# Fused attention and two expert layers: layer two of a token tile issued behind layer one of the next tile, and all transposes of a tile in one block of 64-row turns

## The reference

```python
def _moe2_ref(x, w_gate, w_output_gate, w1, w2):
    logits = x @ w_gate
    e_idx = np.argmax(logits, axis=1)
    ...
    for e in range(E):                      # E = 8
        mask = e_idx == e
        if not mask.any():
            continue
        h = np.maximum(x[mask] @ w1[e], 0.0)      # 512 -> 1024
        ye = h @ w2[e]                            # 1024 -> 512
        out[mask] = gate_w[mask, None] * eom[mask, e, None] * ye
```

## Time and profile before

| | |
|---|---|
| runs | 889.3, 894.98, 890.36 us; median 890.36 |
| the profiled execution | 894.22 us, of which the span from the first to the last instruction is 892.5 us |
| busy share of the span | PE 96%, DVE 43%, ACT 29%, POOL 18% |
| mean granted TensorE clock | 0.991 of full speed |
| chain that ended last | PE 90%, DVE 3%, issue 3%, DMA 2% |

### The profile page before, as it was taken

How to read it: one execution, slowest core, us unless ns; L and a number is a source line. 1 busy time by engine, 2 the same in 40 slices (tenths; PEclk the granted TensorE clock), 3 DMA queues, 4 the chain that set the end, 5 groups by cost and what they waited for, 6 DMA issues and landing times.

```text
span 892.5 us, 18919 instructions
## 1 busy us (share of the span) xinstructions
PE 857.6 (96%) x7096; PEld 720.9 (81%) x7097; DVE 385.5 (43%) x770; ACT 257.1 (29%) x387; POOL 163.7 (18%) x223
## 2 busy tenths in 40 slices
PE   8998998999999999999999999998989999999994
PEld 6897897888888888888888888987768888888883
DVE  5786895211133322334223341467765224534431
ACT  4564453111131112211131111325243113323311
POOL 5775300700000000000000000000133333322321
PEclk9999998999999999999999999999999999999997
DMA  9885733500020000200020000106611116106100
GB/s 260 241 245 171 234 119 104 154 1 0 1 95 1 1 1 0 94 0 0 0 71 0 0 0 0 49 1 213 213 50 46 47 35 221 55 35 229 40 25 18
DMA packets 51301, 68.54 MB, mean 77 GB/s; under 512 B 9774, under 2 KB 36014, under 8 KB 51248
## 3 DMA queue, kind: packets, MB, share of 16 engines
q1 hardware_dynamic: 44400, 45.20, 15.9%
q0 software_dynamic: 6560, 22.56, 7.9%
q10 hardware_dynamic: 288, 0.02, 0.0%
HBM read 54.11 MB, written 14.70 MB: 77 GB/s over the span
## 4 chain that ended last, share of the span: by engine, by line
PE 90%; DVE 3%; issue 3%; DMA 2%; ACT 1%; SPq 0%; DVEq 0%; ACTq 0%; POOL 0%; POOLq 0%
PE bank L1347 32%; PE bank L1366 15%; PE bank L1544 11%; PE bank L1572 11%; PE bank L1318 4%; PE bank L1236 4%; PE bank L1263 4%; PE bank L1559 2%; PE bank L1300 1%; PE bank L1376 1%; PE bank L1509 1%; PE bank L1418 1%; PE bank L1337 1%; DMA xg<-y_rows,early_rows 1%; DMA k_sb<-kT 1%
## 5 line engine op out<-in xcount | busy, mean ns | idle before, releaser
L989 DVE TENSOR_TENSOR prod<-silu,bank 128x512 f32<-128x512 f32 x48 | 33.0, 686 | 182.9 <-PE bank L1347 182.9
L1347 PE MATMUL bank<-x_hi,wg_hi 128*128 128x512 f32 (+1 forms) x240 | 91.5, 381 | 0.0
L1347 PE MATMUL bank<-x_hi,wg_lo 128*128 128x512 f32 (+1 forms) x240 | 88.5, 369 | 0.0
L1347 PE MATMUL bank<-x_lo,wg_hi 128*128 128x512 f32 (+1 forms) x240 | 88.4, 368 | 0.0
L1347 PE MATMUL bank<-x_hi,wv_hi 128*128 128x512 f32 (+1 forms) x240 | 88.3, 368 | 0.0
L1347 PE MATMUL bank<-x_lo,wv_hi 128*128 128x512 f32 (+1 forms) x240 | 88.3, 368 | 0.0
L1347 PE MATMUL bank<-x_hi,wv_lo 128*128 128x512 f32 (+1 forms) x240 | 88.3, 368 | 0.0
L517 POOL DMA_INDIRECT xg<-y_rows,early_rows x2 | 3.0, 1522 | 430.2 <-DVE early_rows L947 429.9
L641 ACT ACTIVATE silu<-bank 128x512 f32<-128x512 f32 x48 | 28.7, 598 | 179.6 <-PE bank L1347 179.6
L1366 PE MATMUL bank<-wo_hi,h_hi 128*128 128x512 f32 x192 | 75.5, 393 | 0.0
L1366 PE MATMUL bank<-wo_hi,h_lo 128*128 128x512 f32 x192 | 74.8, 390 | 0.0
(11 more groups left out here) (244 smaller groups left out, 1621.5 us busy)
## 6 DMA issues: line engine op xcount, KB each, us to landing
e_w<-w SPq DMA_DIRECT2D x32, 512.0 KB, 6.0
stage<-w_out POOLq DMA_DIRECT2D x16, 384.0 KB, 3.9
y_rows<-y_sb SPq DMA_DIRECT2D x18, 256.0 KB, 2.1
k_sb<-kT SPq DMA_DIRECT2D x16, 256.0 KB, 4.9
v_sb<-v SPq DMA_DIRECT2D x16, 256.0 KB, 4.7
q_sb<-qT SPq DMA_DIRECT2D x16, 256.0 KB, 3.5
x_rows<-x_sb SPq DMA_DIRECT2D x16, 256.0 KB, 4.1
x_in<-x_rows SPq DMA_DIRECT2D x4, 1024.0 KB, 5.7
```

The costliest lines, as they stand in the source:

```text
L989: dve.tensor_tensor(both(prod[:]), both(silu[:]), bank[V_BANK][:], ALU.mult).then_inc(prod_ready, 1)
L1347: mm = pe.matmul(acc[:, 0:width], w[:, k, cols], x[:, k, 0:width], start=(k == 0 and i == 0), stop=(k == KC - 1 and i == 2))
```

## The change

Five things change in the expert layer and in its run-up.

1. **The shift.** In PE's loop, layer one of tile `t` is followed by layer two of tile `t-1`. Layer two of the last tile stands behind the loop.
2. **One block of turns.** Between steps 3 and 4 of that layer two, PE transposes all of `h_sb` of tile `t` and the rows of tile `t+1`, in 24 transposes of 64 rows (upper and lower half alternating, into different banks) in place of 12 of 128 rows. Before step 3 it waits for the ReLU and for the gathered rows (`turnable`).
3. **Wider operations.** ACT does the ReLU of all 1024 columns in one operation, and `hT_hi`; DVE `hT_lo`; each 1024 columns wide. DVE's scaling of tile `t-1` (`scaled_ahead`) stands behind `hT_lo` of tile `t`, and `hT_hi` of tile `t` waits until layer two of tile `t-1` is done, since `hT_hi` is a single buffer.
4. **The run-up.** Routing steps of the 256-token group go one or two steps `c` earlier or later; tile 1 gets its own row buffer, so both early gathers are issued together; `choose_first` and `early_places` come earlier.
5. **The tables.** Columns first (`col_ready`), the rest after; `hT_lo` of tile 1 goes ahead of the table; the turn of tile 2's rows goes from step 6 to step 2 of tile 1's layer two; POOL looks up tile 1's scale before it gathers tile 2.

PE:

```diff
             layer2(1, 0, 0, 1)
             turn_h(1, 1)
-            layer2(1, 0, 1, 6)
+            layer2(1, 0, 1, 2)
             turn_rows(2)
-            layer2(1, 0, 6, EC)
+            layer2(1, 0, 2, 4)
...
-            with pe.Fori(2, tiles) as t:
-                rank = pe.value_load(table[0:1, bass.ds(t + T_RANK, 1)], min_val=0, max_val=E - 1)
...
+            def turnable(t):
+
+                pe.wait_ge(ha_ready, t + 1)
+                pe.wait_ge(xg_in, (t + 1) * 16)
+
+            def turn_halves(t):
+
+                for c in range(EC):
+                    for a in range(2):
+                        rows = slice(a * TAIL, (a + 1) * TAIL)
+                        mm = pe.transpose(bank[2 + a][:, c * TAIL:(c + 1) * TAIL], h_sb[rows, c * P:(c + 1) * P], ident[rows, rows])
+                mm.then_inc(ht_done, 1)
...
+            first_layer(2)
+            layer2(1, 0, 4, 5)
+            turnable(2)
+            layer2(1, 0, 5, 6)
+            turn_halves(2)
+            layer2(1, 0, 6, EC)
+            with pe.Fori(3, tiles) as t:
+                first_layer(t)
+                rank = rank_of(t - 1)
+                second_layer(t - 1, rank, 0, EC // 2 - 1)
+                turnable(t)
+                second_layer(t - 1, rank, EC // 2 - 1, EC // 2)
+                turn_halves(t)
+                second_layer(t - 1, rank, EC // 2, EC)
+            second_layer(tiles - 1, rank_of(tiles - 1), 0, EC)
```

ACT and DVE:

```diff
+            def h_high_halves(t):
+
+                act.wait_ge(ht_done, t + 3)
+                act.wait_ge(l2_done, alone(act, t + 1))
+                act.activation(by_halves(hT_hi[:]), h_halves(), ACT.Copy).then_inc(hthi_ready, 1)
+
             with act.Fori(2, tiles) as t:
-                relu(t, 0)
-                h_high(t, 0)
-                rows_high(t + 1)
-                h_high(t, 1)
+                relu_all(t)
+                rows_high_halves(t + 1)
+                h_high_halves(t)
                 share(t)
...
+            def scaled_ahead(u):
+
+                dve.wait_ge(l2_done, u + 1)
+                dve.wait_ge(ro_ready, alone(dve, u))
+                dve.wait_ge(sc_in, u * 16)
+                dve.tensor_scalar(o_sb[:], bank[7][:], scale_in[:, 0:1], None, ALU.mult).then_inc(o_ready, 1)
+
+            rows_low_halves(3)
+            h_low_halves(2)
+            share(2)
+            with dve.Fori(3, tiles) as t:
+                rows_low_halves(t + 1)
+                h_low_halves(t)
+                scaled_ahead(t)
                 share(t)
-                scaled(t)
+            scaled_ahead(tiles)
```

POOL:

```diff
-            early_gather(0)
+            for t in range(TT):
+                early_gather(t)
             pool.wait_ge(early_at_ready, 1)
             pool.wait_ge(scale_out, 16)
             scale_lookup(scale_early, EARLY * P, early_at[:, 0:1])
-            pool.wait_ge(xt_done, 1)
-            early_gather(1)
             scatter(0, early_rows[:, 0:1])
+            scale_lookup(scale_early, EARLY * P, early_at[:, 1:2])
...
             gather_ahead(0)
-            tiles = pool.value_load(table[0:1, T_TILES:T_TILES + 1], min_val=1, max_val=SLOTS)
+            gather_ahead(1)
+            scatter(1, early_rows[:, 1:2])
...
-            with pool.Fori(1, tiles) as t:
+            with pool.Fori(2, tiles) as t:
                 tile(t)
```

More of the change, by code:

```diff
@@ L171, in build @@
         e_lo = sb("e_lo", [P, 2 * CH * CW], F32R)
[L172 to L175, removed]
+        xg, xg_second = stage[:, 0, 0:DM], stage[:, 1, 0:DM]
+        xgT_hi, xgT_lo = (sb(n, [P, KC * P], F32R) for n in ("xgT_hi", "xgT_lo"))
+        hT_hi, hT_lo = (sb(n, [P, EC * P], F32R) for n in ("hT_hi", "hT_lo"))
         h_sb = sb("h_sb", [P, EF])
-        hT_lo = sb("hT_lo", [P, EC * P], F32R)
         o_sb = sb("o_sb", [P, DM])
@@ L847, in route_at @@
             def route_at(g):
-                return (4, 5, 0) if isinstance(g, int) and g == NG - 1 else (R_BANK, R_BANK, 256)
+                return (4, 5, 0) if isinstance(g, int) and g in (NG - 3, NG - 1) else (R_BANK, R_BANK, 256)
             def choose(g, base):
@@ L1137, in _ @@
+            col_t = of_tile(t1[:], shift_e[:], te2)
+            then(next(col_t),
+                 dve.memset(table[0:1, T_COL + SLOTS:T_COL + 32], 0))
+            then(next(col_t))
+            dve.tensor_tensor(table[0:1, T_COL:T_COL + SLOTS], t1[0:1, :], iota_f[0:1, 0:SLOTS], ALU.add
+                              ).then_inc(col_ready, 1)
+            then(dve.tensor_tensor(ee2[:], earlier[:], over_tiles(used_e[:], E), ALU.mult),
                  dve.tensor_tensor(e1[:], used_e[:], iota_f[:, 0:E], ALU.mult),
@@ L1138, in _ @@
                  dve.tensor_tensor(e3[:], used_e[:], base_e[:], ALU.mult))
-            then(dve.tensor_tensor(te_in[:], te_in[:], te1[:], ALU.mult),
+            then(dve.tensor_reduce(rank_e[:], ee2[:], AX.X, ALU.add))
+            scaled(0)
+            rank_t = of_tile(t_rank[:], rank_e[:], te1)
+            then(next(rank_t),
+                 dve.tensor_tensor(ee1[:], over_experts(iota_f[:, 0:E], E), over_tiles(rank_e[:], E), ALU.is_equal))
+            h_low(1, 0)
+            then(next(rank_t),
@@ L1615, in _, with second_layer @@
                 layer1(t, rank, 0, 0, KC)
-                layer1(t, rank, 1, 0, 2)
-                turn_h(t, 0)
-                layer1(t, rank, 1, 2, KC)
-                turn_rows(t + 1)
-                layer2(t, rank, 0, 1)
-                turn_h(t, 1)
-                layer2(t, rank, 1, EC)
+                layer1(t, rank, 1, 0, KC)
+            def second_layer(t, rank, k0, k1):
+                if k0 == 0:
+                    pe.wait_ge(elo_ready, rank * CH + CH)
+                    pe.wait_ge(ht_ready, t + 3)
+                    pe.wait_ge(o_ready, t + 1)
+                for k in range(k0, k1):
+                    at = slice(k * P, (k + 1) * P)
+                    for i, (h, w) in enumerate(((hT_hi, e_hi), (hT_hi, e_lo), (hT_lo, e_hi))):
+                        mm = pe.matmul(bank[7][:], h[:, at], w_part(w, rank, HALF_W + k * DM),
+                                       start=(k == 0 and i == 0), stop=(k == EC - 1 and i == 2))
+                if k1 == EC:
+                    mm.then_inc(l2_done, 1)
```

136 lines of the change are left out of this document (80 added, 56 removed).

## The result

The changed kernel took 951.94 us (median of 4 runs, 948.09 to 955.23) against 892.0 for the kernel before on the same chip (4 runs, 889.3 to 894.98): a ratio of 1.0676, 95% interval 1.0631 to 1.0721. It is 60 us slower; 954 was forecast. The profiled execution took 954.31 us, 2.4 above its median, with a span of 952.5. PE is busy for 92% of it (near 90% was forecast).

A forecast was written before the change was run, and what follows sets the result against it. PE alone bounded the loop before; the gather's chain would bound it after. 666.3 + 12.1 + 232 + 6 and 6 + 10 + 23.5 gave a 956 us span, 957.7 with surroundings; profiling's 3.9 off, 954 us, range 925 to 982.

The forecast's parts named there:

- The chain: Loop: layer two, `hT_hi`, `hT_lo`, `o_sb`, scatter, gather make the turn 14.5 us; +2.2 us in sixteen turns, +35 us.
- The block of turns: PE's 24 transposes a turn take 1.2 us against 1.4, between 0.9 and 1.4; PE alone needs 12.1 us a turn.
- The landing: Loop: a gather lands 3.4 us after its start, a price taken from the earlier profile's row of this transfer.
- The estimate of 2.6 us: Skill's formula for a gather of 262,144 bytes, 0.8 us below the row; would lower the sum by 13 us.
- The loads: Two turns with weight loads: gather takes 6.4 us instead of 3.4, +6 us in all; ACT's splits add nothing.
- The clock: Loop waits: 3 of 14 turns have a fall at 3.2 us, +10 us, bounds 0 and 14; load turns +6.
- The run-up: Ahead of the loop: layer one of tile 3 starts at 666.3 us instead of 671.07, -4.8, one layer two still owed.
- The end: Behind the loop nothing covers the last tiles' `hT_lo` and `o_sb`: 23.5 us against 12.9.
- That the chain is shorter than 7.5 us: Rival, loop: rows land before PE's 34th matmul, PE needs 12.1 us a turn; 890 us median, chance 0.09.
- That the clock holds: Rival: no fall of the clock in any wait, the sum without 10, 6 and 3; 935 us, chance 0.26.
- That it falls in nearly every turn: Rival, loop: eleven more falls of the clock, 35 us; 989 us, chance 0.13.

The follow-up runs named there:

- e1_pool: Changed kernel with POOL issuing the gather of the tile after next ahead of the scatter: 904.26 us, ratio to before 1.0145.
- e2_scale_first: Changed kernel with DVE scaling `o_sb` ahead of making `hT_lo`: 910.8 us, ratio to before 1.0213.
- e4_dose: Changed kernel with one more DVE operation of the shape of `o_sb` just ahead of it in every turn: 969.77 us, ratio to before 1.0871.
- e3_turns128: Changed kernel with twelve turns of 128 rows for the 24 of 64, copies over whole banks: 961.03 us, ratio to before 1.0782.
- e12_late_alone: Changed kernel with the table starting the splits of weights one turn later, POOL's order unchanged: 956.63 us, ratio to before 1.0747.
- e5_fill: Changed kernel with ten unused bf16 matmuls on PE just ahead of its two waits in the turn: 945.08 us, ratio to before 1.0611.
- e6_pool_runup: e1_pool, with tile 2's gather also ahead of tile 0's scatter and the second scale lookup in the run-up: 904.91 us, ratio to before 1.0171.
- e11_rows_first: e10_all with DVE making `xgT_lo` of tile 2 ahead of the table of the splits' turns: 891.9 us, ratio to before 1.0017.
- e10_all: e6_pool_runup with weight splits one turn later for experts of three tiles or more, and `o_sb` ahead of `hT_lo`: 890.31 us, ratio to before 1.0006.

## Why the prediction was right, point by point

**The chain.** Right in mechanism and in size. Forecast from the start of a turn: `hT_lo` 2.5, `o_sb` 3.2, scatter 4.2, gather 6.4, landing 9.8, turn 14.5. The trace has 2.55, 3.20, 4.09, 6.19, 9.6 and 14.39. e1_pool and e2_scale_first take its two halves away, e4_dose lengthens it, and the turn follows each time. PE alone needs the 12.0 us of e1_pool (12.1 forecast), so an undisturbed turn of 14.39 is 2.4 us longer than PE's own work. PE's waits in the sixteen turns are 40.6 us, 38 forecast. That these are so near is partly luck: the forecast put 2.4 us into each, and the trace has 29.6 us in the fourteen ordinary turns, 2.1 each, and 5.7 and 5.3 in the load turns.

**The block of turns.** It takes 0.99 us, not 1.2, near the lower of my bounds (0.9); before, the twelve turns took 12.28 - 10.9 = 1.4 us. The Trainium skill, TensorEngine Tiling (Array Packing), section Key Properties, says that a change of mode drains TensorE. No row shows the drain by itself; whatever it costs is inside these 0.99 us. It does not cost more than the 64-row turns win: e3_turns128, without the change of mode, is 0.24 us a turn slower. The gain of 12.28 - 12.0 = 0.3 us a turn is real, and it only shows when the chain is out of the way.

**The landing.** 3.2 to 3.5 us in thirteen of the fourteen ordinary turns and 2.65 in one. The row was the right price. The estimate of 2.6 us from the Trainium skill, DMA: Bandwidth & Descriptors, section Anatomy of one DMA — SWDGE (gpsimd) path, is too low for this transfer, and would have made the forecast 13 us lower.

**The loads.** Forecast +6 for the slow gather in two turns and +6 for the clock; measured 20.4 - 14.4 = 6.0 us in each, 12 in all. The landing beside a load was 7.0 and 6.7 us, not 6.4. The sentence that ACT's splits end about when the gather lands and add nothing was right (e12_late_alone), but behind it stood a second wait of nearly the same size, which e1_pool uncovers. One thing was not forecast: in the turn behind a load the gather starts 2.8 us behind the scatter and not 2.1, 0.7 us more in each of the two.

**The clock.** That the sum was right is luck, two errors that cancel. Forecast 3 falls of 3.2 us (+10); there were 6, at 1.5 us each, 9 us, of which e5_fill gives back 8.4. The price was taken from the one long stretch of the earlier trace rows, where the low clock lasted 6.7 us and not 3.5. Of turns with the same wait of 2.1 us some have a fall and their neighbours none; what decides is not shown.

**The run-up.** Layer one of tile 3 was forecast 4.8 us earlier; it is 5.4 earlier counted from the first gate product. Both waits of 4.6 and 1.6 us stand where they were forecast (5 and 1.7). The fall of the clock between them was priced too high here too: the granted clock is 0.79 from 648 to 656 us, 8 x 0.21 = 1.7 us for the 3.2 forecast. The forecast named only POOL's order as the cause of the first wait: e6_pool_runup and e11_rows_first show that DVE's table and ACT's splits stand at the same place.

**The end.** +10.6 us was forecast behind the loop, and 11.4 came: the loop's last matmul starts at 927.99, so the loop ends 0.23 later, at 928.22, and from there it is 24.3 us to the end of the span, against 23.5 forecast and 12.9 before. The other 2 of the 13.5 us lie in tile 19's own turn, which the chain makes longer than a turn of before; the forecast had them in the loop's sixteen. The 0.8 us too little is a term of the sum: tile 19's scale lookup was forecast at 8.7 us behind the loop and starts at 10.0, since the copies ahead of it wait until the scatter of tile 18 has landed, and DVE's last scaling waits for the lookup:

```profile
937.02 0.18 POOL L573 COPY row_out<-place_rows 128x1 uint32 x1 [1.56 <-DMA out<-o_sb,row_out]
938.18 1.02 POOL L532 DMA_INDIRECT scale_in<-scale_rows,scale_row  x1 [0.86 <-POOL scale_row L574]
940.34 0.75 DVE L1248 TENSOR_SCALAR o_sb<-bank,scale_in 128x512 f32<-128x512 f32 x1 [8.93 <-DMA scale_in<-scale_rows,scale_row]
```

**The rivals.** That the chain is shorter than 7.5 us is excluded by sixteen waits. That the clock holds would have been 935: e5_fill, in which it holds in the ordinary turns only, is at 945, and the forecast less its 10 us for them is 944. That it falls in nearly every turn did not happen; e4_dose, with 0.66 us more of waiting, comes close, with ten of thirteen.

## What to carry to other kernels

When a loop is shifted so that a result is asked for earlier in the turn, add up the chain that must produce it within the turn, over all engines and in their order, and compare it with the work of the waiting engine up to that point; here 9.8 us against 7.5, and moving one operation on DVE was worth 41 us, moving one on POOL 48. What such a shift wins (0.3 us a turn in cheaper transposes) is paid at the end, where nothing covers the last tile: with all the waits in the loop gone it was worth nothing. In e10_all the run-up is 4.2 us shorter than before, the loop 3.5 and the end 8.0 us longer. The run-up's gain is no gain: one layer two (5.4 us) is put off from it to the end, so apart from that the run-up is 1.2 us longer and the end 2.6. Two waits that end together must be taken away together before either experiment says anything, and ahead of the loop there were three.

## What the runs showed of the hardware

- With waits of about 2 us (1.3 to 2.9) in every turn of 14 to 17 us the granted clock fell to near its lower level in 6 of 14 turns, for some 3.5 us and at 1.5 us each, which is shorter than the 6.7 us seen in the earlier trace rows; behind waits over 5 us it stayed low for 7 us. With bf16 matmuls in those waits it did not fall in the ordinary turns, and from tile 3 to tile 19 the kernel was 6.2 us faster for doing more (its median is 7 us lower, but the intervals of the two ratios overlap).
- 24 turns of 64 rows, with the change of form ahead and behind, are faster than 12 of 128 rows that carry the same data: 0.99 against 1.23 us.
- A gather that starts beside a load of 8 chunks lands in 6.7 to 7.0 us and not in 3.4. In the two turns behind such a load the scatter's issue on POOL took 1.64 and 1.65 us for 1.01, and the turn without a fall of the clock was 0.7 us longer than others (15.13 for 14.39).
- Ahead of the first gate product, code that is the same in all kernels took from 146.2 to 155.8 us in the twelve traces.
